# One more pass of two first-FFN blocks in groups of 15 block products, and nine weight sums made during the groups

## The chip, the cores and the metric

The kernel runs on one core of a Trainium2 chip. The metric is the device time of the whole program in microseconds. TensorE (PE) multiplies, VectorE (DVE) and ScalarE (ACT) work on SBUF and PSUM, GpSimd (POOL) on SBUF alone, and SyncE (SP) issues all the DMAs.

## What is computed

```python
# q, k, v, f_logit: 4 batches, 8 heads, 768 tokens, head_dim 48
f = 1 / (1 + exp(-f_logit))
for t in range(768):
    state = f[t][:, None] * state + outer(k[t], v[t])
    y[t] = q[t] @ state
x = y as 3072 tokens x 384
x = ((x @ w_a) * (x @ w_b)) @ w_out          # first FFN, d_ff 1536
p = domain_probs / (sum(domain_probs) + 1e-9)
out = sum over 4 experts e of p[:, e] * (relu(x @ w1[e]) @ w2[e])   # second FFN, d_ff 1024 each
```

## The kernel before

The 3072 tokens are eight blocks of TB1 = 384. Every float32 matmul is made from three: each operand is split into a rounded half (hi, made by ACT) and a rest (lo, made by VectorE or GpSimd), and hi x hi, lo x hi and hi x lo are added up in PSUM (`three`, L2577).

**Attention** is 32 units (a pair of heads, 384 tokens). Units 0 to 3 run alone at the start. Each of the others goes through limit, logs (exp and ln), sums (a scan), decays, inverses, ends, gates (GpSimd), keys, turn (transposes), krt, kv and scores (TensorE), mask and state (VectorE), output (TensorE) and y (ACT). The table `J` (L110) says at which part j of the plain FFN a unit's turn stands; the offsets of `TOGETHER` and its kin (L112) place its other steps. Units 8 to 31 are six parts apart.

**The first FFN, plain.** Blocks 0 to PLAIN - 1 = 5. One step i is one of 12 slices of d_ff of one block and has three parts: up_1(i, 0), up_1(i, 1) and down_1(i - 1), each of nine 384-column matmuls. ACT does a_out(i) and h_round(i), VectorE gate(i) and h_rest(i). Four loops over j in range(3 * N1) write out the order of TensorE, ACT, VectorE and GpSimd; SP has a fifth.

**Groups.** The other two blocks of the first FFN, and all of the second FFN, take two blocks (768 tokens) in a pass. The product of a 3 x 3 block matrix of weights (FG = 3 tiles of d_ff, 3 of d_model) with 3 x 2 blocks of x is made from 15 block products instead of 18 (`R`, `MADE`, `CHAINS`). For it, 11 sums of x blocks are made for each pass (x2_sum on VectorE, sum_hi on ACT, sum_lo on GpSimd), and 11 sums of weight blocks for each set of weights: w_sum(q, 0 to 15) on GpSimd, out of a buffer that load_w1(q) fills, and stored to DRAM by store_sums(q) (`weight_sums`). There are NS = 18 sets: 8 for the first FFN and 10 for the second. In a group, SP loads the set's 15 blocks (load_wu), ACT and GpSimd split them (up_round, up_rest), TensorE makes the products (up_2), ACT and VectorE copy and add the chains (copy, add), and h is made, split and multiplied down (h1_round, h1_rest or h2_round, h2_rest; down_round, down_rest; down) and added to the result (weigh). A pass of the first FFN is 8 groups, in turn one for a and one for b; a pass of the second is a small group of 2 tiles and ten full ones. The order inside a group is written out by hand for each engine; where passes change, three groups are written as one piece (`turned`, L534), since the next pass's x operands are made there.

All 18 weight sets are made during the plain blocks: w_sum(q) at parts SUMS_AT + SUMS_PACE * q (L163), with the loads and stores in SP's queue between the loads of the units. SP works its queue in order: an issue whose semaphore isn't there yet holds all that stand behind it. The buffer of x2_sum is a ring of NXT = 8 (2 for the first pass).

The lines that the prediction's steps touch: PLAIN (L40), `J` (L110), the sets' pace (L163), x2_sum's ring (L281, L1870), load_w1 (L791), store_sums, load_wd (L844), the SP loop over groups, turn (L2473), scores, kv and output, w_sum (L1522), product (L2695), down (L2779).

Of the kernel before, what the change touches and what calls it, by code (L numbers as in the profile page):

```python
# [7 lines left out]
def gated_attention_then_two_ffns(nc, fkq, v, vT, probs, wa, wb, wo, w1, w2, out):  # L8
# [31 lines left out]
    PLAIN = 6  # L40
# [10 lines left out]
    NS = 2 * NF + NQ  # L51
    TT = 2 * TB1 // 128
# [57 lines left out]
    J = {u: 5 * (u - FIRST) + 8 if u < 2 * PPB else 6 * (u - FIRST) + 5 for u in range(FIRST, NU)}  # L110
# [8 lines left out]

    FIRST_OF_2 = dict(CLOSE, logs=-7, sums=-6, decays=-5, ends=-4)  # L120
# [3 lines left out]
               for step, after in (FIRST_OF_2 if u == FIRST else SECOND_OF_2 if u == FIRST + 1 else LAST_OF_2 if u == 2 * PPB - 1 else CLOSE if u < 2 * PPB else  # L124
                                   LAST_OF_ALL if u == NU - 1 else TOGETHER).items()}
# [37 lines left out]
    SUMS_AT, SUMS_PACE = 31, 9  # L163
    WU_AT, WD_AT = (3 * FT1 * (PLAIN - 1) + 18, 3 * FT1 * (PLAIN - 1) + 32), 3 * FT1 * (PLAIN - 1) + 29

    def x2_at(n):
        return CMIN_AT + 9 + 2 * n
# [6 lines left out]
    with perm:  # L174
# [106 lines left out]
        NXT = 8  # L281
# [12 lines left out]

        for n in range(12, NX):
            x_operand(n)
# [378 lines left out]
        def x2_free(eng, p, o):  # L675
# [5 lines left out]
            elif n < 8 or n == 11:  # L681
                attention_done(eng)
            else:
                eng.wait_ge(s_upb, FT1 * (PLAIN - 1) + max(0, (n - 10) // 2))

# [25 lines left out]
        def w1_raw(f, k):  # L711
            return raw.rearrange("p a n -> p (a n)")[:, (k * FG + f) * 128:(k * FG + f + 1) * 128]
# [42 lines left out]
        def _(eng):  # L755
# [35 lines left out]
            def load_w1(q):  # L791
# [5 lines left out]
                dst = raw.rearrange("p a n -> p (a n)")[:, 0:KT * FG * 128].rearrange("p (k f) -> p k f", k=KT)  # L797
# [46 lines left out]
            def load_wd(g):  # L844
                if downs(g) == 0:
                    eng.wait_ge(s_ws, 16 * NS)
# [55 lines left out]
            for j in range(3 * N1):  # L902
# [14 lines left out]
                for q in range(NS):  # L917
                    if j == SUMS_AT + SUMS_PACE * q + 6:
                        if q + 1 < NS:
                            load_w1(q + 1)  # L920
                        store_sums(q)
                    if j == SUMS_AT + SUMS_PACE * q + 4:
# [9 lines left out]
            for g in range(G):  # L932
# [86 lines left out]
        def _(eng):  # L1019
            eng.preload_act_table_set("natural_log_exp_and_others")  # L1020

            def logs(u):
                t = unit_ring[ring(u)][0:P2, F, :]
                eng.wait_ge(s_lim, u + 1)
                eng.activation(t, t, ACT.Exp, scale=-1.0).then_inc(s_exp, 1)
                eng.wait_ge(s_exp, u + 1)
# [119 lines left out]

            logs(0)
            logs(1)
            decays(0)
            inverses(0)  # L1150
            decays(1)
            logs(2)
            inverses(1)
            logs(3)
# [23 lines left out]
            for j in range(3 * N1):  # L1178
                if j == STRONG_AT:
                    flag = is_strong(eng)  # L1180
                i, part = j // 3, j % 3
# [1945 lines left out]
```

## Time and profile before

| | |
|---|---|
| time, median of 3 runs | 1293.82 us (1293.12 to 1294.21) |
| the profiled execution | 1291.46 us, of it the span 1289.7 us |
| TensorE busy, matmul / weight load | 1280.1 / 1258.5 us |
| VectorE, ACT, GpSimd busy | 915.8, 635.5, 684.1 us |
| granted TensorE clock | 1.00 |

The stages by time: units 0 to 3 to about 28 us, plain blocks with attention to 380 us, plain blocks alone to about 440 us, the grouped pass of the first FFN to about 552 us, four passes of the second FFN to the end. "Busy" of an engine is the time covered by its instructions; a matmul's recorded 0.33 us overlaps the next one's. In the rows below, a time in brackets is how long the engine stood before the instruction, and the arrow names what let it go.

### The profile page before, as it was taken

To read this page: it belongs to the slowest core of one execution; us is meant where nothing else is said; L and a number is where in the kernel's file an instruction comes from. 1 tells how busy PE (TensorE), PEld (TensorE's weight loads), DVE (VectorE), ACT (ScalarE), POOL (GpSimd) and SP (SyncE) were. 2 spreads that over 40 slices of the span, in tenths; PEclk is the share of its full clock that TensorE was granted. 3 is DMA by queue.
4 is the path that set the end of the run, shared out by engine and by line. 5 is a ranking of instruction groups with operands and counts; after the bars stand their busy time and mean duration, and the time that the engine had idled before them with its cause. 6 is when DMAs were issued, how large, how long until landed. Compare 5 with 4: busy or idle time off the path is not lost.

```text
span 1289.7 us, 26428 instructions
## 1 busy us (share of the span) xinstructions
PE 1280.1 (99%) x9319; PEld 1258.5 (98%) x9319; DVE 915.8 (71%) x1775; ACT 635.5 (49%) x1316; POOL 684.1 (53%) x739
## 2 busy tenths in 40 slices
PE   9999999999999999999999999999999999999999
PEld 7999999999999989999999999999999999999998
DVE  8866766767645478767887677787668777677765
ACT  7654444445434455644444554445554455544442
POOL 4336766657656466574444744444744444644440
PEclk9999999999999999999999999999999999999999
DMA  8524445553433143132332242232342332432221
GB/s 258 171 75 147 138 137 153 157 163 117 130 98 128 56 124 93 61 109 87 98 99 81 83 145 83 86 99 61 104 137 85 98 92 66 138 110 87 82 86 38
DMA packets 90324, 140.59 MB, mean 109 GB/s; under 512 B 8848, under 2 KB 64336, under 8 KB 90192
## 3 DMA queue, kind: packets, MB, share of 16 engines
q1 hardware_dynamic: 90192, 138.89, 35.4%
q8 instruction: 76, 1.25, 0.4%
q14 instruction: 56, 0.46, 0.1%
HBM read 119.98 MB, written 22.41 MB: 110 GB/s over the span
## 4 chain that ended last, share of the span: by engine, by line
PE 97%; DVE 1%; DMA 0%; issue 0%; POOL 0%; ACT 0%; SPq 0%; DVEq 0%; ACTq 0%; POOLq 0%
PE bank L2809 10%; PE bank L2810 10%; PE bank L2808 10%; PE bank L2578 10%; PE bank L2580 9%; PE bank L2579 9%; PE bank L2708 6%; PE bank L2706 6%; PE bank L2707 6%; PE score_banks L2708 3%; PE score_banks L2706 3%; PE score_banks L2707 3%; PE bank L2568 2%; PE bank L2572 2%; PE score_banks L2497 1%; PE score_banks L2526 1%
## 5 line engine op out<-in xcount | busy, mean ns | idle before, releaser
L1576 POOL TENSOR_TENSOR wu<-w_r,wu 128x640 fp32r<-128x640 f32 (+1 forms) x156 | 242.4, 1568 | 96.2 <-ACT wu L1084 96.2
L1581 POOL TENSOR_TENSOR wd<-raw,wd 128x384 fp32r<-128x384 f32 x140 | 142.3, 1030 | 272.5 <-ACT wd L1089 272.5
L2120 DVE SCALAR_TENSOR_TENSOR xt<-bank,pn,xt 128x384 f32<-128x384 f32 x288 | 176.8, 615 | 148.7 <-PE bank L2810 143.9
L2808 PE MATMUL bank<-wd,h_hi 128*128 128x384 f32 x768 | 257.6, 335 | 0.0
L2809 PE MATMUL bank<-wd,h_hi 128*128 128x384 f32 x768 | 257.5, 335 | 0.0
L2810 PE MATMUL bank<-wd,h_lo 128*128 128x384 f32 x768 | 257.4, 335 | 0.0
L2708 PE MATMUL bank<-x_lo,wu 128*128 128x384 f32 x479 | 161.5, 337 | 0.0
L2706 PE MATMUL bank<-x_hi,wu 128*128 128x384 f32 x479 | 160.3, 335 | 1.0 <-DVE hb L2025 1.0
L2707 PE MATMUL bank<-x_hi,wu 128*128 128x384 f32 x479 | 160.3, 335 | 0.0
L2578 PE MATMUL bank<-xs_hi,wab 128*128 128x384 f32 x426 | 148.2, 348 | 0.4 <-ACT a_sb L1135 0.4
L2809 PEld LDWEIGHTS bank<-wd,h_hi 128*128 128x128 f32 x768 | 144.2, 188 | 0.0
L2808 PEld LDWEIGHTS bank<-wd,h_hi 128*128 128x128 f32 x768 | 144.2, 188 | 0.0
L2810 PEld LDWEIGHTS bank<-wd,h_lo 128*128 128x128 f32 x768 | 144.1, 188 | 0.0
L2579 PE MATMUL bank<-xs_hi,wab 128*128 128x384 f32 x426 | 142.7, 335 | 0.0
L2580 PE MATMUL bank<-xs_lo,wab 128*128 128x384 f32 x426 | 142.6, 335 | 0.0
L1105 ACT ACTIVATE h<-bank 128x384 f32<-128x384 f32 x144 | 67.6, 489 | 131.7 <-PE bank L2708 131.5
L1084 ACT ACTIVATE wu<-w_r 128x640 fp32r<-128x640 f32 (+1 forms) x156 | 105.7, 706 | 25.4 <-PE bank L2708 7.6
L2706 PEld LDWEIGHTS bank<-x_hi,wu 128*128 128x128 f32 x479 | 89.9, 188 | 1.4 <-DVE hb L2025 1.4
L2708 PEld LDWEIGHTS bank<-x_lo,wu 128*128 128x128 f32 x479 | 89.9, 188 | 0.0
L2707 PEld LDWEIGHTS bank<-x_hi,wu 128*128 128x128 f32 x479 | 89.9, 188 | 0.0
L1124 ACT ACTIVATE h_hi<-h 128x384 fp32r<-128x384 f32 x120 | 61.7, 521 | 45.3 <-DVE h L2045 42.2
L2578 PEld LDWEIGHTS bank<-xs_hi,wab 128*128 128x128 f32 x426 | 79.9, 188 | 2.6 <-ACT a_sb L1135 0.7
(253 smaller groups left out, 2871.5 us busy)
## 6 DMA issues: line engine op xcount, KB each, us to landing
w_r<-weight_sums SPq DMA_DIRECT2D x144, 320.0 KB, 2.9
raw<-w SPq DMA_DIRECT2D x48, 576.0 KB, 4.0
unit<-fkq SPq DMA_DIRECT2D x28, 504.0 KB, 4.6
weight_sums<-w_s SPq DMA_DIRECT2D x18, 384.0 KB, 4.5
v_in<-v_chunks SPq DMA_DIRECT2D x32, 144.0 KB, 4.2
out<-xt SPq DMA_DIRECT2D x24, 192.0 KB, 4.3
weight_sums<-w_s SPq DMA_DIRECT2D x54, 64.0 KB, 4.0
weight_sums<-w SPq DMA_DIRECT2D x40, 64.0 KB, 2.7
```

Of the source, the lines that this page charges most:

```text
L1576: eng.tensor_tensor(wu_piece(g, n, 1), wu_raw(g, n), wu_piece(g, n, 0).bitcast(f32), ALU.subtract).then_inc(s_ulo, 1)
L1581: eng.tensor_tensor(wd[half(g)][:, 1, n, :], wd_raw(n), wd[half(g)][:, 0, n, :].bitcast(f32), ALU.subtract).then_inc(s_dlo, 1)
L2120: eng.scalar_tensor_tensor(out=acc(b, t), in0=d, scalar=w, in1=acc(b, t), op0=ALU.mult, op1=ALU.add).then_inc(s_acc, 1)
L2578: eng.matmul(o, w_hi, m_hi, start=start, stop=False)
L2579: eng.matmul(o, w_lo, m_hi, start=False, stop=False)
L2580: return eng.matmul(o, w_hi, m_lo, start=False, stop=stop)
L2706: eng.matmul(to, w_hi, x_hi, start=start, stop=False, skip_group_check=True)
L2707: eng.matmul(to, w_lo, x_hi, start=False, stop=False, skip_group_check=True)
L2708: eng.matmul(to, w_hi, x_lo, start=False, stop=True, skip_group_check=True).then_inc(s_step, 1)
L2808: eng.matmul(o, hh, w_hi, start=(f == fs[0]), stop=False)
L2809: eng.matmul(o, hh, w_lo, start=False, stop=False)
L2810: mm = eng.matmul(o, hl, w_hi, start=False, stop=(f == fs[-1]))
```

## The change

- PLAIN goes from 6 to 4: blocks 4 to 7 of the first FFN are grouped, in two passes (groups 0 to 7 and 8 to 15); the groups of the second FFN are 16 to 59.
- The 28 later units of attention share 48 plain steps instead of 72. `J` spaces units 8 to 31 by 3.65 parts for SP; on the four other engines the loops over j are replaced by lists written out call by call. exps is taken out of logs, and exp and ln of a unit are placed apart.
- Sets 0 to 8 of the weight sums are made in the plain blocks (NSA = 9, pace 10), sets 9 to 17 in groups 2, 4, 6 to 8, 10, 14 to 16, 17, 18, 19 and 20, out of a new buffer raw_s. Its room comes from x2_t (NXT 8 to 5).
- load_w1 and store_sums for these sets stand in SP's loop over the groups, behind the group's load_wu and load_wd.
- scores waits for the states of the units before it, output(31) for the evacuation of unit 30.
- The order inside the groups is written anew, on all engines.

```diff
-    PLAIN = 6
+    PLAIN = 4
...
+    NSA = 9
...
-    J = {u: 5 * (u - FIRST) + 8 if u < 2 * PPB else 6 * (u - FIRST) + 5 for u in range(FIRST, NU)}
+    J = {u: 5 * (u - FIRST) + 8 if u < 2 * PPB else 29 + (u - 2 * PPB) * 365 // 100 for u in range(FIRST, NU)}
...
-    SUMS_AT, SUMS_PACE = 31, 9
+    SUMS_G = (2, 4, 8, 10, 14, 17, 18, 19, 20)
+    SUMS_AT, SUMS_PACE, SUMS_LONG = 31, 10, 8
...
-        NXT = 8
+        NXT = 5
...
+        raw_s = sb(later, "raw_s", [128, KT * FG * 128])
...
-            p, q = GROUPS[g]
-            after = 2 * NF if PASSES[p][0] == 1 else NQ
-            return q == after - 1 and p + 1 < len(PASSES) or q == NQ and p > 0
+            return any(r[0] < g <= r[-1] for r in ((14, 16), (6, 8), (25, 27), (36, 38), (47, 49)))
...
-                    eng.wait_ge(s_ws, 16 * NS)
+                    eng.wait_ge(s_ws, 16 * NSA)
...
+                if g + 1 in SUMS_G:
+                    q = NSA + SUMS_G.index(g + 1)
+                    if q > NSA:
+                        store_sums(q - 1)
+                    load_w1(q)
+                elif g == SUMS_G[-1]:
+                    store_sums(NS - 1)
...
+                    up_rest(g + 2, 2)
                     product(g + 1, 1)
                     product(g + 1, 2)
...
+                    for n in range(0, 4):
+                        w_sum(11, n)
                     sum_lo(p + 1, 6)
                     sum_lo(p + 1, 7)
                     sum_lo(p + 1, 8)
                     sum_lo(p + 1, 9)
                     sum_lo(p + 1, 10)
...
+                elif g == 18:
+                    up_rest(g + 1, 0)
+                    up_rest(g + 1, 1)
+                    up_rest(g + 1, 2)
+                    down_rest(g, 0)
+                    down_rest(g, 1)
+                    down_rest(g, 2)
+                    for n in range(0, 16):
+                        w_sum(15, n)
...
                 if u >= FIRST:
+                    eng.wait_ge(s_st, states(u, 0))
...
+                if u == NU - 1:
+                    eng.wait_ge(s_ys, NU - 1)
...
-            for j in range(3 * N1 - 2):
...
+            up_1(24, 1)
+            turn(20)
+            kv(20)
+            scores(20)
+            output(19)
+            down_1(23)
+            up_1(25, 0)
+            turn(21)
+            up_1(25, 1)
+            output(20)
+            kv(21)
...
```

## Rows read from the trace of the kernel before

**Rows 1.** The page's first part: busy time, share of the span, instructions of TensorE.
```profile
PE 1280.1 (99%) x9319; PEld 1258.5 (98%) x9319; DVE 915.8 (71%) x1775; ACT 635.5 (49%) x1316; POOL 684.1 (53%) x739
```
**Rows 2.** The page's chain of work that ended last, by engine.
```profile
PE 97%; DVE 1%; DMA 0%; issue 0%; POOL 0%; ACT 0%; SPq 0%; DVEq 0%; ACTq 0%; POOLq 0%
```
**Rows 3.** Stretches: length, then busy PE, PEld, DVE, ACT, POOL; clock, DMA, GB/s.
```profile
30.00:380.00 350.00, 349.30 (x3888) 332.82 (x3888) 235.54 (x487) 168.28 (x344) 208.49 (x329) 1.00 0.46 137
452.00:556.00 104.00, 101.10 (x578) 100.17 (x577) 80.04 (x158) 57.45 (x120) 66.66 (x54) 1.00 0.32 97
640.00:760.00 120.00, 120.00 (x692) 120.00 (x691) 88.43 (x167) 61.28 (x132) 64.81 (x54) 1.00 0.32 97
```
**Rows 4.** Timeline of PE, first groups: start, duration, instruction, [stood before it, releaser].
```profile
454.92 0.44 PE L2706 MATMUL bank<-x_hi,wu 128*128 128x384 f32 x1 [1.04 <-DVE hb L2025]
465.17 0.42 PE L2578 MATMUL bank<-h_hi,wd 128*128 128x384 f32 x1 [1.86 <-DVE h_lo L2073]
```
**Rows 5.** Timeline of PE in a full group, 27 matmuls apart.
```profile
700.15 0.33 PE L2808 MATMUL bank<-wd,h_hi 128*128 128x384 f32 x1
...
704.83 0.34 PE L2808 MATMUL bank<-wd,h_hi 128*128 128x384 f32 x1
```
**Rows 6.** The page's costliest groups: line, operation, count, busy us, mean ns.
```profile
L2808 PE MATMUL bank<-wd,h_hi 128*128 128x384 f32 x768 | 257.6, 335 | 0.0
```
**Rows 7.** Timeline of PE: output of two units in turn, and one turn.
```profile
161.72 0.86 PE L2568 MATMUL bank<-att,v_in 128*48 128x128 f32 x12
...
173.88 0.86 PE L2568 MATMUL bank<-att,v_in 128*48 128x128 f32 x12
...
205.17 0.45 PE L2481 MATMUL bank<-ident,kr 112*128 112x112 f32 x3
205.39 0.42 PE L2578 MATMUL bank<-xs_hi,wab 128*128 128x384 f32 x1
205.65 0.34 PE L2579 MATMUL bank<-xs_hi,wab 128*128 128x384 f32 x1
```
**Rows 8.** Timeline of ACT: the copy of a unit's transposes.
```profile
205.66 0.45 ACT L1046 ACTIVATE krt<-bank 128x336 f32<-128x336 f32 x1
```
**Rows 9.** h_rest and gate by line: count, duration ns min/median/max, first and last start.
```profile
L1862 DVE TENSOR_TENSOR h_lo<-h_sb,h_hi x72: 544/558/1941, 32.9 to 443.1; 128x384 fp32r<-128x384 f32 x72
L1858 DVE TENSOR_TENSOR h_sb<-a_sb,bank x72: 542/554/556, 31.1 to 441.9; 128x384 f32<-128x384 f32 x72
```
**Rows 10.** Two stretches of 10 us, columns as in rows 3.
```profile
40.00:50.00 10.00, 10.00 (x100) 9.62 (x99) 8.99 (x17) 7.61 (x14) 5.22 (x4) 1.00 0.78 225
50.00:60.00 10.00, 10.00 (x126) 9.50 (x125) 9.23 (x19) 6.20 (x12) 1.62 (x2) 1.00 0.38 112
```
**Rows 11.** Timeline of DVE: mask of a unit, first and last operation of its state.
```profile
200.54 1.22 DVE L1785 COPY_PREDICATED att<-causal,score_banks 64x384 f32<-64x384 int32 x2 [2.77 <-PE score_banks L2497]
...
204.68 0.20 DVE L1834 COPY st_in<-score_banks 112x48 f32<-112x48 f32 x1
...
206.12 0.26 DVE L1836 SCALAR_TENSOR_TENSOR st_carry<-st_in,cend,score_banks 112x48 f32<-112x48 f32 x1
```
**Rows 12.** Stretch, instructions that touch w_s alone: length, POOL busy (count).
```profile
30.00:380.00 350.00, 131.63 (x258) 1.00 0.46 137
```
**Rows 13.** up_rest, down_rest and sum_lo by line, columns as in rows 9.
```profile
L1576 POOL TENSOR_TENSOR wu<-w_r,wu x156: 733/1587/2002, 415.7 to 1249.1; 128x640 fp32r<-128x640 f32 x144, 128x256 fp32r<-128x256 f32 x12
L1581 POOL TENSOR_TENSOR wd<-raw,wd x140: 1003/1022/1379, 431.3 to 1264.2; 128x384 fp32r<-128x384 f32 x140
L1512 POOL TENSOR_TENSOR x_lo<-x_t,x_hi x55: 1004/1019/1336, 394.6 to 1108.4; 128x384 fp32r<-128x384 f32 x55
```
**Rows 14.** One issue of SP in the chain; DMA issues: count, KB each, us to landing.
```profile
1.28 0.42 SPq L767
...
raw<-w SPq DMA_DIRECT2D x48, 576.0 KB, 4.0
```
**Rows 15.** Waits: who for whom, us in total, times, longest.
```profile
POOL w_s L1535 <- DMA weight_sums<-w_s: 86.0, 17, 8.3
```

More of the change, by code:

```diff
@@ L118, in gated_attention_then_two_ffns @@
     LAST_OF_ALL = dict(TOGETHER, output=8, y=9, store=10)
+    NEAR = dict(load=-9, v=-4, limit=-6, logs=-5, sums=-5, decays=-4, gates=-3, ends=-3, keys=-2, turn=0, krt=1, scores=2, kv=2, mask=3, state=4, output=6, y=7, store=8)
     FIRST_OF_2 = dict(CLOSE, logs=-7, sums=-6, decays=-5, ends=-4)
@@ new lines, in _ @@
+            first_lo(9)
+            gate(4)
+            first_lo(10)
+            h_rest(4)
+            first_lo(11)
+            first_lo(12)
+            first_lo(13)
+            first_lo(14)
+            gate(5)
+            ends(6)
+            keys(6)
+            sums(7)
+            limit(8)
+            limit(9)
+            h_rest(5)
+            mask(5)
+            probs(0)
+            state(5)
+            ends(7)
+            sums(8)
+            first_lo(15)
+            gate(6)
@@ new lines, in _ @@
+            h_rest(6)
+            keys(7)
+            mask(6)
+            state(6)
+            ends(8)
+            first_lo(16)
+            sums(9)
+            keys(8)
+            gate(7)
+            mask(7)
+            state(7)
+            limit(10)
+            first_lo(17)
+            h_rest(7)
+            ends(9)
+            gate(8)
+            keys(9)
+            h_rest(8)
+            sums(10)
+            limit(11)
+            mask(8)
+            state(8)
+            ends(10)
@@ new lines, in _ @@
+            gate(9)
+            h_rest(9)
+            sums(11)
+            ends(11)
+            keys(10)
+            gate(10)
+            mask(9)
+            state(9)
+            h_rest(10)
+            gate(11)
+            h_rest(11)
+            keys(11)
+            probs(1)
+            limit(12)
+            limit(13)
+            mask(10)
+            gate(12)
+            state(10)
+            sums(12)
+            h_rest(12)
+            ends(12)
+            sums(13)
+            y_out_1(0)
@@ new lines, in _ @@
+            mask(11)
+            state(11)
+            gate(13)
+            limit(14)
+            h_rest(13)
+            keys(12)
+            gate(14)
+            ends(13)
+            sums(14)
+            keys(13)
+            ends(14)
+            h_rest(14)
+            mask(12)
+            state(12)
+            gate(15)
+            probs(2)
+            probs(3)
+            limit(15)
+            keys(14)
+            h_rest(15)
+            mask(13)
+            state(13)
+            limit(16)
@@ new lines, in _ @@
+            mask(21)
+            state(21)
+            ends(23)
+            keys(23)
+            h_rest(26)
+            mask(22)
+            state(22)
+            gate(27)
+            sums(24)
+            h_rest(27)
+            mask(23)
+            state(23)
+            limit(25)
+            gate(28)
+            limit(26)
+            ends(24)
+            keys(24)
+            h_rest(28)
+            sums(25)
+            sums(26)
+            ends(25)
+            keys(25)
+            mask(24)
@@ L2019, in add @@
+            x2_sum(0, 9)
+            gate(46)
+            plain_lo(0, 3)
+            x2_sum(0, 10)
+            h_rest(46)
+            gate(47)
+            h_rest(47)
+            flag = is_strong(eng)
             def add(g, n):
```

2060 lines of the change are left out of this document (1527 added, 533 removed).

## Prediction

> **What bounds the kernel now.** I read the page from the top. TensorE is busy for 1280.1 of 1289.7 us [rows 1], and the chain that ended last runs through it for 97% of the span [rows 2]. So the time is the number of matmuls times their distance, plus the few places where TensorE stands. The table of stretches says where those are: from 30 to 380 us (attention beside the first FFN's plain blocks) TensorE stands 0.7 us, from 640 to 760 us not at all, and from 452 to 556 us (the one pass of grouped first FFN) 2.9 us, the others at start and end [rows 3]. The 2.9 us are two single waits: 1.04 us before the fifth product of group 1, for an add, and 1.86 us before the first down product of group 1, for h_lo [rows 4]. VectorE and GpSimd are far from full in these stretches, 67% and 60% in the attention stretch, 77% and 64% at most in the groups [rows 3]. They can't shorten anything, but they can become late.
>
> **Matmuls removed.** A matmul of 384 columns starts 4.68 us / 27 = 0.1733 us after the one before it [rows 5], at a granted clock of 1.00 (the level of 2.4 GHz) in every stretch of rows 3, in the groups and in the plain blocks alike; I use 0.1735 us. A plain block has 12 steps of up_1 (a and b, 3 k, 3 halves: 18) and down_1 (3 tiles, 3 halves: 9), so 324 matmuls, and two blocks 648. The same two blocks as one pass of groups: 8 groups of 15 products of 3 matmuls, 360, and 4 down parts of 6 tiles, 3 f and 3 halves, 216, together 576. 72 matmuls less: 72 x 0.1735 = **12.5 us** off TensorE. The second FFN keeps all of its own, among them the 3 x 768 of its down products [rows 6].
>
> The Trainium skill, "TensorE: Matmul & The Clock Gate", section "Back-to-back issue gap", gives N/2.4 + 2.5 ns for an isolated gap, 162.5 ns at 384 columns, and the saving by it would be an estimated 11.7 us. The same section says that streams with weight loads do better than that at 512 columns; rows 5 show worse than the formula at 384 columns and the rule is not borne out here.
>
> **Attention, moved closer together.** The 28 later units used to be spread over 58 of 72 steps; the order written out now ends with output(31) after up_1(39, 0), 522 matmuls or 90.6 us sooner. Their own matmuls stay. A unit costs TensorE 173.88 - 161.72 = 12.16 us less 54 x 0.1735, so 2.8 us [rows 7]. A switch to small matmuls and back loses time: the three transposes at 205.17 take 0.22 us to the next weight-heavy matmul, which in turn is followed after 0.26 us and not 0.17 [rows 7]. I put a switch at 0.1 to 0.15 us. Before there are 58 such switches after the first four units; in the new order I count 49, since turn(u + 1) often stands right behind scores(u). 9 x 0.11 = **1.0 us** saved; bounds 0 and 1.5.
>
> Against this stand new waits. One is written in: turn(20) is followed at once by kv(20), which needs ACT's copy of the transposes. The copy takes 0.45 us [rows 8], and with a hop before and behind it TensorE stands **0.8 us** (bounds 0.45 and 1.2), and nothing else is queued to cover it. In all other units at least a down_1 or an up_1 (1.56 us) lies between the two.
>
> The other is VectorE's load. From 30 to 380 us it is busy 235.5 us [rows 3]. 58.5 steps of gate and h_rest at 2 x 0.55 us [rows 9] are 64 us, the splits of late weights and probs some 13, and the rest is 28 units at 5.6 us. Now the same 28 units share 350 - 91 = 259 us with 19.3 steps less: 235.5 - 21 = 214 us, so 83% of the stretch, up from 67%. It is uneven. Between gate(25) and gate(29) VectorE has four units and four steps, 22.4 + 4.4 = 26.8 us, and TensorE has 108 matmuls and three units, 18.7 + 8.4 = 27.1 us: 99%. Between gate(5) and gate(9) it is about as full, with seven weight and unit items in front. Between gate(29) and gate(37) it falls to 70%. In the old kernel VectorE ran 90% and 92% full in two slices of 10 us with TensorE at 10.00 of 10.00 [rows 10], so high load alone costs nothing there. At 99% it does; I take **1.5 us**, bounds 0 and 8.
>
> The round trip is what makes it sharp. output(u) waits for mask(u) and state(u), 1.22 us and 1.7 us on VectorE [rows 11], 2.9 us together, counted from scores(u). Before, six parts of a step (9.4 us) lay between scores and output. In the new order seven units (6, 7, 12, 15, 21, 24, 27) have only turn and two parts, 3.6 us, and five more have 4.4 to 4.6 us. The slack of such a unit is 0.7 us, and whatever VectorE is late beyond that TensorE waits.
>
> **Weight sums moved.** A set is 16 GpSimd operations. 258 of them take 131.6 us [rows 12], so a set is 8.2 us. Nine of 18 sets leave the plain blocks and go into groups 2 to 20, into a buffer of their own, raw_s, whose room comes from x2_t (8 buffers to 5). GpSimd has room in the first of these: two groups of the first FFN are 144 matmuls or 25 us, and hold six up_rest at 1.59, three down_rest at 1.02 [rows 13] and two products of about 1.05, so 14.7 us, 22.9 with a set. In groups 17 to 20 (99 matmuls, 17.2 us) it holds 7.8 + 8.2 = 16.0 us: 93%. The sums stand last in each list, and up_rest of the next group is wanted a whole group later, so I cost them at nothing. If that cover goes, each us of lateness is a us.
>
> At one place the cover seems too short. At the pass change of groups 6 to 8, w_sum(11, 0 to 3) stands ahead of sum_lo(6 to 10). Its data comes by load_w1(11), which SP issues only after load_wu(9) and load_wd(9) and the five stores of set 10, behind up_rest(8, 2). Eight issues of 0.42 us and a landing of 4.0 us [rows 14] are 7.4 us after up_rest(8, 2); GpSimd has two products (2.1 us) to do meanwhile and then stands with five sum_lo behind the wait. Counted from the start of group 7: up_rest(8, 2) ends at about 11.9 (1.0 until the first piece is there, three up_rest 4.8, six sum_lo 6.1 [rows 13]), the data is there at 19.3, sum_lo(6) ends at 22.3. Group 8's ninth product, which reads it, stands after 15 + 8 products and 5 down tiles, 114 matmuls or 19.8 us. TensorE stands **2.5 us**; bounds 0 and 4. In the old kernel GpSimd waited 86 us in 17 places for such stores and loads, up to 8.3 us [rows 15], none of it felt by TensorE, which speaks for the lower bound.
>
> The two waits of rows 4 stay: the lines of group 0 on ACT and of TensorE around group 1 are the same (y_out and three up_round ahead of copy(1, 0)). I cost the reorder at nothing, bounds -2 and +1. The pass change that is new (first FFN to first FFN) is three groups of 36 us; 30 adds, 11 sums, 4 plain_lo and some 17 other operations at 0.5 us are 31 us on VectorE, 86%, and I put it at nothing, bounds 0 and 2. New waits before scores (s_st) and before output(31) are for things that kv and the order have waited for already: nothing.
>
> **Sum.** -12.5 - 1.0 + 0.8 + 1.5 + 2.5 = -8.7 us. The profiled execution took 1291.46 us, so 1282.8 by it; the median of the runs is 2.36 us above it, so **1285.1 us**.
>
> **Rivals.**
> (a) The whole gain: the lists hide everything but kv(20), and one wait of group 1 goes. -12.5 - 1.0 + 0.8 - 1 = -13.7: 1280. For it: in the groups of the old kernel, which are written out in the same manner, TensorE never stands from 640 to 760 us [rows 3].
> (b) VectorE is the bound in the two full stretches. Its operations with two SBUF inputs stretch beside GpSimd: h_lo has 558 ns as the median and 1941 at most, while h_sb, with one input in PSUM, never exceeds 556 [rows 9]. With more packed into less time 27 us at 99% become 110%, twice or three times: 6 to 8 us more than I took, 1291. The Trainium skill, "SBUF — State Buffer", section "Who interferes with whom", has the pair of ports as an exclusive lock: by that rule the second to come waits a whole instruction. Rows 9 agree.
> (c) GpSimd is late in the groups: at 93%, with its operations stretched by the same contention (640-wide ones to 2002 ns [rows 13]), groups 17 to 20 and the two pass changes lose about 1.5 us each: 9 us on top of none from the attention, 1290.
> (d) Slower: the round trip scores, mask, state, output sets the pace of the attention. With two units in flight a late mask delays output, evacuation and the next turn. It decides against the change from 13.5/28 = 0.48 us of standing per unit on; at 0.65 us per unit it is 18 us and 1298. For it: a slack of 0.7 us in seven units. Against it: units with 8 to 15 us of room stand between, in which VectorE catches up.
>
> **Chances.** Forecast (1282 to 1288) 0.45; (a) 0.21; (b) 0.12; (c) 0.08; (d) 0.14. A measurement of this kernel can tell 0.2%, or 2.6 us. (b) and (c) end at 1288 to 1295, a little over half of them below 1291.2, so faster 0.77, same 0.09, slower 0.14. The range reaches over (a), (b) and (c), from 1279.0 to 1295.0, and leaves (d) out.
>
> **What would show it.** The count of 384-column matmuls down by 72. TensorE's idle time by stretch: under 1 us from 640 us on; up to 3 us before up_2(8, 8) with GpSimd at w_sum waiting for a DMA; 0.8 us at kv(20), with ACT's krt as releaser; a few tenths at L1785 or L1836 as releasers where units come in pairs. (b) would show as masks or gates as releasers around gate(5 to 9) and gate(25 to 29); (c) as up_rest or sum_lo; (d) as state before most outputs. Wrong altogether would be a longer distance of matmuls, or a clock below 1.00 after new waits.

## The result and the profile after

The kernel after takes 1362.87 us (median of 4 runs, 1353.32 to 1364.68), the kernel before 1293.47 us beside it (1292.65 to 1294.21). The ratio is 1.052, 95% interval 1.047 to 1.057: **5.2% slower**, where 1285.1 us was forecast, and 68 us beyond the top of the range.

The page's first part, and the chain of work that ended last, of after:

```profile
PE 1298.8 (95%) x9247; PEld 1267.3 (93%) x9247; DVE 971.8 (71%) x1884; ACT 662.5 (49%) x1373; POOL 723.7 (53%) x788
...
PE 68%; POOL 5%; issue 2%; DMA 2%; DVE 2%; SPq 1%; ACT 1%; DVEq 0%; ACTq 0%; POOLq 0%
```

TensorE has 9247 matmuls where it had 9319 [rows 1]: the 72 are gone, as counted. Yet it is busy 18.7 us longer and stands 64.2 us of the span of 1363.0, where it stood 9.6. The chain went through TensorE for 97% [rows 2], now for 68%. Three stretches of after, with the columns of rows 3:

```profile
30.00:330.00 300.00, 270.30 (x3263) 249.74 (x3267) 193.84 (x437) 136.94 (x294) 127.18 (x193) 0.95 0.42 122
360.00:700.00 340.00, 313.19 (x1720) 307.44 (x1719) 247.08 (x438) 161.81 (x336) 249.91 (x294) 0.96 0.38 118
700.00:1300.00 600.00, 600.00 (x3453) 600.00 (x3452) 450.53 (x844) 306.69 (x632) 297.20 (x243) 1.00 0.32 97
```

The attention stretch holds 29.7 us of standing, the groups in which weight sums are made 26.8 us, and behind 700 us there is none. VectorE is busy 65% in the first and 73% in the second: idle time of TensorE beside idle time of VectorE means that both wait. The granted clock was 0.95 and 0.96, where it was 1.00 everywhere in rows 3. Six of the larger stands (one of 4.68 us, at 69.50, is the largest of the attention), from TensorE's timeline (start, duration, instruction, [stood before it, releaser]), and two of the waits (who for whom, us in total, times, longest):

```profile
206.56 0.66 PE L3442 MATMUL bank<-h_hi,wo_hi 128*128 128x384 f32 x1 [4.35 <-DVE h_lo L2390]
...
441.79 0.69 PE L3805 MATMUL score_banks<-x_hi,wu 128*128 128x384 f32 x1 [2.46 <-DVE hb L2831]
...
487.15 0.69 PE L3805 MATMUL score_banks<-x_hi,wu 128*128 128x384 f32 x1 [3.55 <-DVE h L2831]
...
533.72 0.59 PE L3805 MATMUL score_banks<-x_hi,wu 128*128 128x384 f32 x1 [3.49 <-DVE hb L2831]
...
634.69 0.69 PE L3805 MATMUL score_banks<-x_hi,wu 128*128 128x384 f32 x1 [6.06 <-DVE h L2867]
...
689.47 0.44 PE L3907 MATMUL bank<-wd,h_hi 128*128 128x384 f32 x1 [3.21 <-DVE xt L2926]
```
```profile
DVE unit L2249 <- DMA unit<-fkq: 45.0, 18, 6.5
...
POOL w_s L1882 <- DMA raw_s<-w: 30.0, 4, 8.8
```

**The sum.** By my working TensorE should have stood 9.6 us plus 0.8 + 1.5 + 2.5 = 14.4 us, and been busy 1280.1 - 12.5 - 1.0 = 1266.6 us. It stood 64.2 (+49.8) and was busy 1298.8 (+32.2). These 82.0 us are the difference between the span of the profiled execution, 1363.0 us, and the 1281.0 us that the working gives for one.

**The busy time** grew mostly because TensorE ran at the lower of its two clock levels (1.2 GHz) about its longer stands. Its timeline behind the stand of 2.46 us:

```profile
442.59 0.52 PE L3807 MATMUL score_banks<-x_lo,wu 128*128 128x384 f32 x1
442.91 0.52 PE L3805 MATMUL bank<-x_hi,wu 128*128 128x384 f32 x1
443.23 0.52 PE L3806 MATMUL bank<-x_hi,wu 128*128 128x384 f32 x1
...
445.14 0.34 PE L3806 MATMUL bank<-x_hi,wu 128*128 128x384 f32 x1
445.32 0.34 PE L3807 MATMUL bank<-x_lo,wu 128*128 128x384 f32 x1
```

Matmuls of 384 columns start 0.32 us apart and, some 3 us later, 0.18. At full clock it is 0.1733 [rows 5]; ten of them at 0.32 cost 1.5 us more. The granted clock of after was 0.50 in twelve stretches, eight of 3.4 us and four of 6.8, and TensorE was busy for 49.5 us in them. By an estimate from that, half of those 49.5 us, 24.8, is the most that the clock can have cost of the 32.2.

The other 7.4 us or more have another cause. The kernel mended (experiment 10) has 3.4 us at the lower level and is still busy for 1277.1 us, only 3.0 less than before, where the working had 13.5 less. A stand costs busy time beyond its own length: the last matmul ahead of it counts its whole 0.33 us, of which the next one otherwise overlaps 0.16, and the first one behind it comes 0.28 us before the next and not 0.17. TensorE stands for 0.05 us or more in 8 places before, in 43 in after and in 37 in mended. At 0.27 us each that is some 9 and 8 us, an estimate which no run here tests.

**The attention.** Where does VectorE wait? Before 206.56 its timeline has limit(u), which takes the logits of a unit, and h_lo, which TensorE wants, right behind it:

```profile
205.52 0.36 DVE L2249 TENSOR_SCALAR unit<-unit 112x384 f32<-112x384 f32 x1 [3.58 <-DMA unit<-fkq]
205.79 0.16 DVE L2268 COPY cend<-dec 112x6 f32<-112x6 f32 x1
205.87 0.55 DVE L2390 TENSOR_TENSOR h_lo<-h_sb,h_hi 128x384 fp32r<-128x384 f32 x1
```

The data is late, and VectorE, which works its list in order, can't go past it. When was it asked for? The end of output(u - 4) on TensorE, SP's issue of the next unit, and limit, in one of the cases:

```profile
212.91 0.22 PE L3436 MATMUL bank<-unit,st_in 48*48 48x64 f32 x2
...
213.17 0.34 SPq L766 DMA_DIRECT2D unit<-fkq  x1
...
217.86 0.36 DVE L2249 TENSOR_SCALAR unit<-unit 112x384 f32<-112x384 f32 x1 [0.52 <-DMA unit<-fkq]
```

The issue comes 0.26 us behind the last matmul that reads the old unit, the data 4.7 us after it. A unit's buffer is one of a ring of four, and load(u) waits for s_y of unit u - 4. Units are 3.65 steps apart, so y(u - 4) stands at J(u) - 14.6 + 7 = J(u) - 7.6, behind the step written for the load, -9. A step takes 1.56 us of plain matmuls and 2.8 / 3.65 us of a unit's, about 2.3 us without any stand. So the 4.7 us are 2.0 steps, the data is there at about -7.6 + 2.0 = -5.6 at the best, and limit(u) stands at -6. In the kernel before the same sum was -24 + 10 = -14 against a limit at -10: 4 steps of room. That is my theory of the ring, found only after the first experiments.

### The profile page after: what moved, and what is told of

Read it like the earlier page. It is cut to its first block, busy times and chain, and to the rows that moved or that the text cites. A ratio compares the mean times of both kernels' runs of the same rounds, so it can differ in the third digit from the quotient of the medians.

```text
span 1363.0 us, 26767 instructions
## 1 busy us (share of the span) xinstructions
PE 1298.8 (95%) x9247; PEld 1267.3 (93%) x9247; DVE 971.8 (71%) x1884; ACT 662.5 (49%) x1373; POOL 723.7 (53%) x788
## 4 chain that ended last, share of the span: by engine, by line
PE 68%; POOL 5%; issue 2%; DMA 2%; DVE 2%; SPq 1%; ACT 1%; DVEq 0%; ACTq 0%; POOLq 0%
PE bank L3909 10%; PE bank L3908 10%; PE bank L3907 10%; PE bank L3807 6%; PE bank L3805 6%; PE bank L3806 6%; PE score_banks L3805 3%; PE score_banks L3807 3%; PE score_banks L3806 3%; PE bank L3442 3%; PE bank L3444 3%; PE bank L3443 3%; POOL wu L1923 2%; DMA raw_s<-w 1%; SPq L833 1%
## 5 line engine op out<-in xcount | busy, mean ns | idle before, releaser
L1928 POOL TENSOR_TENSOR wd<-raw,wd 128x384 fp32r<-128x384 f32 x152 | 154.5, 1029 | 320.7 <-ACT wd L1108 320.7
L1923 POOL TENSOR_TENSOR wu<-w_r,wu 128x640 fp32r<-128x640 f32 (+1 forms) x180 | 277.1, 1563 | 24.1 <-ACT wu L1103 24.1
L3805 PE MATMUL bank<-x_hi,wu 128*128 128x384 f32 x559 | 190.0, 340 | 4.4 <-DVE hb L2831 1.5
L3807 PE MATMUL bank<-x_lo,wu 128*128 128x384 f32 x559 | 190.2, 340 | 0.0
L3806 PE MATMUL bank<-x_hi,wu 128*128 128x384 f32 x559 | 189.0, 338 | 0.0
L1103 ACT ACTIVATE wu<-w_r 128x640 fp32r<-128x640 f32 (+1 forms) x180 | 122.6, 709 | 70.1 <-PE bank L3807 30.0
L3805 PEld LDWEIGHTS bank<-x_hi,wu 128*128 128x128 f32 x559 | 106.9, 191 | 7.0 <-DVE hb L2831 2.2
L3805 PE MATMUL score_banks<-x_hi,wu 128*128 128x384 f32 x281 | 96.1, 342 | 17.2 <-DVE h L2867 6.8
L3442 PE MATMUL bank<-xs_hi,wab 128*128 128x384 f32 x282 | 101.8, 361 | 10.2 <-DVE h_sb L2386 5.1
L3806 PEld LDWEIGHTS bank<-x_hi,wu 128*128 128x128 f32 x559 | 106.6, 191 | 0.0
L3807 PEld LDWEIGHTS bank<-x_lo,wu 128*128 128x128 f32 x559 | 106.5, 190 | 0.0
L3443 PE MATMUL bank<-xs_hi,wab 128*128 128x384 f32 x282 | 98.2, 348 | 0.0
L3444 PE MATMUL bank<-xs_lo,wab 128*128 128x384 f32 x282 | 97.9, 347 | 0.0
```

The source lines that it names most:

```text
L1923: eng.tensor_tensor(wu_piece(g, n, 1), wu_raw(g, n), wu_piece(g, n, 0).bitcast(f32), ALU.subtract).then_inc(s_ulo, 1)
L1928: eng.tensor_tensor(wd[half(g)][:, 1, n, :], wd_raw(n), wd[half(g)][:, 0, n, :].bitcast(f32), ALU.subtract).then_inc(s_dlo, 1)
L3442: eng.matmul(o, w_hi, m_hi, start=start, stop=False)
L3443: eng.matmul(o, w_lo, m_hi, start=False, stop=False)
L3444: return eng.matmul(o, w_hi, m_lo, start=False, stop=stop)
L3805: eng.matmul(to, w_hi, x_hi, start=start, stop=False, skip_group_check=True)
```

## Experiments

Thirteen kernels. "Standing" is TensorE's in 30:330 and in 360:700; after has 29.7 and 26.8. Experiments 4, 10 and 13 are medians of four runs, all others single runs. The four runs of after lie 11.4 us apart and those of experiment 4 12.9 us, so where two times differ by less than that, the stands in the traces have to tell.

**1. no_sums**: leaves out every weight sum with its loads, copies and stores; the groups multiply by blocks of w1 in place of the sums.

> Leaves out all weight sums with their loads, copies and stores, in the plain blocks and in the groups (the groups multiply by blocks of w1 instead, so the result is not the reference's). Changed kernel: 1363 us, TensorE stands 30 us from 30 to 330 us and 27 us from 360 to 700 us, and works at a lower granted clock behind the stands, some 31 us more of busy time. Theory 1 (queue order): unit loads are late since SP issues sum copies and stores ahead of them, and in the groups up_rest is late since GpSimd's w_sum stands before it waiting for a load: standing falls to under 10 us in the attention stretch and under 5 us in the groups, time 1285 to 1300. Theory 2 (VectorE is the bound at 99% in the full stretches): the attention stretch keeps over 20 us of standing, time 1315 to 1330. Theory 3 (ring of four unit buffers): the same as theory 2 for the attention.

Measured: 1310.97 us, clock 0.996, standing 14.1 and 9.6; VectorE still waits 22.1 us for unit data. So about 52 of the 69 us over before come with the sums, in both stretches, and 17 do not (theory 1 had 1285 to 1300, theory 2 over 20 us of standing: neither came). With no sum at all this kernel is slower than the old one with all of them.

**2. groups_sums_last**: the sums of sets 9 to 13 behind all up_rest and down_rest of a group and none where passes change; load_w1 one group earlier, ahead of the stores.

```
-    SUMS_G = (2, 4, 8, 10, 14, 17, 18, 19, 20)
+    SUMS_G = (1, 3, 5, 9, 11, 13, 17, 18, 19)
...
-                elif g == 4:
-                    for n in range(0, 4):
-                        w_sum(10, n)
-                    up_rest(g + 1, 0)
...
+                elif g in (2, 4, 10, 12):
...
+                    for n in range(8):
+                        w_sum({2: 9, 4: 10, 10: 12, 12: 13}[g], n)
```

> Weight sums 9 to 13 stand behind the up_rest and down_rest of their group on GpSimd, none in the pass changes, and SP issues load_w1 ahead of the five stores of the set before. All else as in the changed kernel. Theory 1 (in the groups GpSimd's list waits for raw_s with up_rest behind it): standing from 360 to 700 us falls from 27 to under 8 us and its share of low clock goes, time 1325 to 1340. Rival (GpSimd's load itself, 16 operations more per set, makes it late): standing stays above 18 us, time above 1350.

Measured: 1342.78 us, standing 28.0 and 13.1, between what the two theories gave. The stands of 2.46 and 3.49 us are gone. So is the one of 3.21 us, and the one of 6.06 is 1.92: these two have a cause of their own, below. This is their chain in after (start, duration, what), for the first of them:

```profile
420.22 0.48 SPq L833
...
424.00 0.45 SPq L815
424.50 4.96 DMA raw_s<-w
429.53 0.46 POOL w_s L1882
...
431.25 1.54 POOL wu L1923
...
433.77 3.09 POOL wu L1923 x2
436.92 2.96 DMA w_r<-weight_sums
440.60 0.48 ACT hb L1124
441.18 0.57 DVE hb L2831
```

SP stores set 9 in five issues, then loads set 10; GpSimd has w_sum(10, 0 to 3) written ahead of up_rest(5, 0) and waits for the load; up_rest is late, so the raw block's buffer, so the next load of blocks, so TensorE.

**3. units_by_act** and **4. both_orders**: ScalarE issues the loads of units 10 to 31 and of v right behind evac_y(u - 4), past SP's queue; 4 has the edit of 2 as well.

```
+            unit_from(eng, 10)
+            v_from(eng, 10)
```

> Units 10 to 31 and their v are loaded from ACT's queue right behind evac_y of the unit that frees the buffer, units 8 and 9 earlier in SP's queue. Groups as in the changed kernel. Theory 1 (loads behind other issues of SP): VectorE's waits for unit data fall from 45 to under 15 us, standing from 30 to 330 us from 30 to under 12 us, time 1320 to 1335. Theory 2 (VectorE is the bound): waits fall but standing stays over 20 us. Theory 3 (four buffers are too few): waits stay over 25 us since the data is asked for at the same output, standing stays over 20 us.

> Both edits together. Theory 1: little standing anywhere, the clock stays at 1.00, and the 72 matmuls show: 1283 to 1295, about 1288, faster than the kernel before by up to 0.8%. Theories 2 or 3 for the attention: 1310 to 1330.

Measured: 1359.73 us, standing 28.1 and 27.9; and 1342.67 us (ratio 1.038, 1.033 to 1.043), standing 29.3 and 16.4. VectorE waited 37.0 and 34.2 us for the data. The theory that SP's long runs of issues made the loads late fell: another queue, and no gain. What both kernels keep is that the load follows output(u - 4).

**5. forget_rows_first**: limit(u) takes only the logits of a unit, and its buffer's row of logits is read for the last time by the key gate, nine steps before output. The row gets a transfer of its own:

```
+            def load_gates(u):
+                eng.wait_ge(s_kg, before_in_ring(u) + 1)
+                eng.dma_start(unit_ring[ring(u)][0:P2, F, :], fkq[pair_of(u), half_of(u), :, F, :])\
+                   .then_inc(s_f[ring(u)], 16)
```

> The kernel after, but from unit 6 on the forget rows of a unit (which limit(u) takes) are loaded by a transfer of their own, as soon as the key gate of unit u-4 has read that row; the key and query rows follow as before, behind output(u-4). One more transfer for each unit on SyncE's queue, the order of every other engine unchanged. Theory ring (limit(u) waits because the unit's buffer is given back only by output(u-4), and its transfer takes 4.5 us more, while the written order has limit(u) 3 steps behind the load): VectorE's wait for unit data falls from 45.0 us to under 10, TensorE's standing in 30:330 from 29.7 us to 10 to 15, time about 1340. Theory VectorE (the shorter spacing simply gives VectorE and the loop scores, mask, state, output too little time): the wait for data falls too, but TensorE stands as before, 25 to 30 us, time 1355 to 1365.

**6. both_and_forget_rows**: with the order of 2 (not 4: the loads stay with SP).

> The same loads with the order of the weight sums in the groups of groups_sums_last. If the two faults are separate, their gains add: theory ring gives 1342.78 less about 20, so some 1320, with 28.0 us of standing in 30:330 falling to 10 to 15; theory VectorE gives 1340 to 1345.

Measured: 1349.1 and 1318.93 us. In 5, wait and stretch:

```profile
DVE unit L2262 <- DMA unit<-fkq: 12.1, 5, 4.4
...
30.00:330.00 300.00, 281.98 (x3446) 260.74 (x3447) 217.10 (x461) 147.43 (x315) 141.57 (x213) 0.99 0.47 134
```

The wait falls from 45.0 to 12.1 us, the standing from 29.7 to 18.0, the clock rises from 0.95 to 0.99, with no order of a computing engine changed. In 6 the standing is 12.1 and 16.3. The gains are 13.8 and 20.1 alone and 43.9 together: 10 us more than their sum, which three single runs against runs 11.4 us apart suggest and do not show. The theory of the ring holds for the 11.7 us of standing (15.9 from experiment 2 to 6), and the rival that VectorE has too little time explains at most what is left. The standing stayed above the 10 to 15 us expected of 5; one of its stands, 3.38 us at 180.29, follows a limit that lasted 6.52 us beside weight sums (below).

**7. no_sums_ring_five**: the kernel of 1 with a fifth buffer and loads at step -11.

> The kernel no_sums (no weight sums, no load, copy or store of them) with a fifth buffer for units from unit 11 on, laid over the region in which the weight sums had their raw weights, and unit loads two steps earlier (at -11). Theory ring: in no_sums VectorE still waited 22.1 us for unit data and TensorE stood 14.1 us in 30:330; with data there early the wait falls under 5 us, the standing to 5 to 9 us, and the time from 1310.97 to about 1304. Theory VectorE: the standing stays at 12 to 15 us and the time at 1310.

Measured: 1310.54 us, standing 10.9 and 10.6; the wait for data falls from 22.1 to 9.3 us. The wait and the standing did not fall as far as expected (under 5 us, and 5 to 9), and the time is the one that the rival gave. Over the whole span TensorE stood 3.2 us less and was busy 2.7 us more (1280.6 for 1277.9), with 13.7 us at the lower clock level for 10.2. So this pair alone does not decide between the two theories. The largest stand left, 3.80 us at 68.6, is that of units 8 and 9, which no later buffer serves.

**8. stands_put_into_before**: TensorE waits in the middle of five full groups for 1, 2, 3, 1 and 5 tiny transfers in turn.

```
+                if g in STANDS and n == 7:
+                    eng.wait_ge(s_stand, 16 * stands_before(g))
```

> The kernel before, with TensorE made to wait in the eighth block product of groups 24, 27, 35, 38 and 46 for 1, 2, 3, 1 and 5 tiny transfers of SyncE one after the other, nothing else changed. It prices a stand of TensorE by itself, with what the granted clock does behind it. Theory clock (the low clock behind a stand is what made TensorE's busy time 31 us longer in the kernel after): stands of 4 us and more are followed by 384-column matmuls 0.32 us apart instead of 0.173 for some us, so that the kernel is longer by clearly more than the sum of the stands, while the short ones cost their own length. Rival (the low clock of the kernel after has another cause, its transfers or its many short idle times): each stand costs its own length, some 2 us for each transfer, 24 us together, and the clock stays at 1.00.

Measured: 1324.98 us, 30.9 over before, with 23.3 us of stands. Stretches (columns as in rows 3) with a stand of one transfer, of two, and behind that of five:

```profile
815.00:825.00 10.00, 7.95 (x46) 7.67 (x46) 5.75 (x11) 2.56 (x6) 4.41 (x4) 1.00 0.31 100
869.00:879.00 10.00, 6.22 (x27) 5.93 (x26) 3.53 (x7) 1.36 (x3) 4.32 (x4) 0.83 0.30 99
...
1212.00:1222.00 10.00, 9.33 (x45) 9.36 (x46) 4.76 (x9) 2.29 (x5) 0.00 (x0) 0.81 0.29 98
```

The two stands of about 2.0 us cost their length and the clock stays at 1.00. Behind 3.78 us, and behind the two longer ones, TensorE runs for 3.2 us at half the clock (ten matmuls at 0.32 us), and then at the full one: 1.5 us each. But the length of a stand does not settle it. The same trace has such a stretch of ten matmuls at two places where nothing was put in, behind stands of 1.66 and 1.85 us:

```profile
31.20 0.58 PE L2589 MATMUL bank<-xs_hi,wab 128*128 128x384 f32 x1 [1.66 <-ACT a_sb L1146]
...
467.89 0.41 PE L2589 MATMUL bank<-h_hi,wd 128*128 128x384 f32 x1 [1.85 <-DVE h_lo L2084]
```

The second of them is the 1.86 us of rows 4, behind which before stayed at full clock. Against the traced run of before (1291.46 us) the kernel is 33.5 us longer: TensorE stands 24.3 us more and is busy 9.3 us more, of which five stretches of ten slow matmuls are 7.5.

**What a run of GpSimd does to VectorE.** In after, two instructions of VectorE lasted 8.27 and 4.12 us. The first, its neighbours, and GpSimd's first and last sum at that time:

```profile
623.99 0.54 DVE L2855 TENSOR_TENSOR h<-h,score_banks 128x384 f32<-128x384 f32 x1
624.46 8.27 DVE L2872 SCALAR_TENSOR_TENSOR h_lo<-h,h_hi 128x384 fp32r<-128x384 f32 x1
632.64 0.55 DVE L2859 TENSOR_TENSOR bank<-h,bank 128x384 f32<-128x384 f32 x1
```
```profile
626.02 0.50 POOL L1882 TENSOR_TENSOR w_s<-raw_s 128x128 f32<-128x128 f32 x1
626.44 0.49 POOL L1884 TENSOR_TENSOR w_s<-raw_s 128x128 f32<-128x128 f32 x1
...
632.38 0.65 POOL L1919 TENSOR_TENSOR w_s<-w_s,raw_s 128x128 f32<-128x128 f32 x1
```

From 620.99 GpSimd goes from one instruction to the next, the sums (sixteen) 0.42 us apart, up to the last, which waits for the one before it and starts 0.07 us behind its end. There VectorE comes in. The Trainium skill, "SBUF — State Buffer", section "Who interferes with whom", says that a VectorE instruction with two SBUF inputs and a GpSimd instruction that reads SBUF exclude each other, and that the loser waits until the other finishes. The trace shows the same pair of instructions, but a wait through 17 GpSimd instructions and not one.

Nor is it confined to two inputs or to the groups. In forget_rows_first limit(u), which reads one tile in SBUF and took 0.36 us above, lasts through a weight sum of the attention, and again up to the gap before the sum's last instruction (VectorE's line, and GpSimd's first, last but one and last):

```profile
171.64 6.52 DVE L2262 TENSOR_SCALAR unit<-unit 112x384 f32<-112x384 f32 x1
...
171.67 0.47 POOL L1893 TENSOR_TENSOR w_s<-raw 128x128 f32<-128x128 f32 x1
...
177.49 0.46 POOL L1927 TENSOR_TENSOR w_s<-w_s,raw 128x128 f32<-128x128 f32 x1
178.03 0.92 POOL L1930 TENSOR_TENSOR w_s<-w_s,raw 128x128 f32<-128x128 f32 x1
```

**9. after_sums_with_gaps**: every weight sum waits for the one before it.

```
+                else:
+                    eng.wait_ge(s_ws, 16 * q + n)
```

> The kernel after; every weight sum on GpSimd now waits for the one before it, so that GpSimd's queue has a gap of some 0.1 us between two of them. Nothing else moves. In the trace of after two VectorE instructions of line 2872 (h_lo from two operands in SBUF, 0.55 us elsewhere) last 8.27 and 4.12 us while GpSimd runs weight sums one right behind the other, and TensorE stands 6.06 and 3.21 us behind them. Theory access (GpSimd's unbroken run keeps VectorE from an operand; a gap lets it in): no VectorE instruction of that line over 2 us between 400 and 700, the stands of 6.06 and 3.21 us gone or under 1 us, each weight sum about 0.1 us longer, time about 1350. Rival (the long record is something else, such as the weight sums' transfers): the long instructions stay and the time is 1360 to 1365.

Measured: 1351.4 us, 11.5 less, which is about as far as the runs of after lie apart. The longest of these instructions between 400 and 700 us are now 3.03 and 2.12 us; of the stands of 6.06 and 3.21 us 0.83 is left. By these stands the theory of access holds, if less purely than I wrote (no such instruction over 2 us).

**10. mended**: 6 with the gaps, with the forget rows of units 8 and 9 ahead of store_x(4), and with this order of ScalarE where passes 0 and 1 change:

```
                     copy(g + 2, 0)
-                    copy(g + 2, 1)
                     h1_round(g + 1, 2)
                     plain_hi(p + 1, 3)
+                    h1_round(g + 1, 3)
...
+                    copy(g + 2, 1)
```

> The kernel both_and_forget_rows with three more edits: every weight sum waits for the one before it; the forget rows of units 8 and 9 are loaded at steps 11 and 12, ahead of the six copies of store_x(4); at the first change of passes ScalarE makes h1_round(7, 2 to 4) and three operands before copy(8, 1) and not behind it. Four stands of TensorE in both_and_forget_rows belong to these: 3.21 us at 67, 3.55 at 454, 2.27 at 607 and 3.45 at 644. By my theories all four go, 12.5 us, and with them some 1.7 us of low clock behind each of three: 1318.9 - 12.5 - 5 = about 1301. If the low clock behind stands were not theirs, 1306; if the third theory is wrong, 1310 or more. The rest to the kernel before would be the small stands of TensorE in the attention.

Measured: **1307.14 us** (ratio 1.011, 1.009 to 1.012), clock 0.998:

```profile
30.00:330.00 300.00, 292.33 (x3516) 271.77 (x3517) 214.53 (x470) 150.44 (x323) 154.93 (x218) 0.99 0.47 138
...
360.00:700.00 340.00, 330.23 (x1881) 325.98 (x1880) 268.12 (x494) 173.41 (x358) 267.02 (x298) 1.00 0.41 131
```

Three of the four stands are gone and the one of 3.55 us is 1.40. 11.8 us came of the 17.5 expected. 55.7 of the 69.4 us by which after is slower are found, each by an edit that moves no work away.

**11. bursts_put_into_before**: sixteen small GpSimd instructions behind down_rest(g, 2) of five late groups; **12. bursts_like_sums**: the same kind of thing in the mended kernel, with the weight sums' own instructions too.

> The kernel before, with 16 small GpSimd instructions added behind down_rest(g, 2) in five full groups: in groups 24 and 35 additions 128x128 of two tiles in SBUF one right behind the other, in 27 and 46 the same with a wait for the one before each, in 38 memsets of 128x128. It shows what a run of GpSimd instructions by itself does to VectorE. Theory access: in 24 and 35 a VectorE instruction with two operands in SBUF lasts several us, until the run ends, and TensorE stands behind it for 2 to 6 us each; in 27 and 46 none is longer than about 1.5 us and TensorE does not stand; in 38 none, as a memset reads nothing. Time 1298 to 1306. Rival (GpSimd's later weight halves are what delays, not VectorE's access): all five groups look the same, and the time is within 2 us of before.

> The kernel mended, with 16 GpSimd instructions added in six full groups behind 700 us: in groups 29, 40 and 43 the sixteen instructions of a weight sum again (operands in the loaded weights, results over the sums, waits as in the kernel after), behind the last, the middle and ahead of the first down_rest; in 32 the same with a wait for the one before each; in 34 and 45 the additions of bursts_put_into_before. Theory access, in the form that is left (an unbroken run keeps VectorE out only at the pace of a weight sum, 0.42 us from start to start, not at the 0.48 us that the additions took): in at least one of 29, 40 and 43 a VectorE instruction with both operands in SBUF lasts over 2 us, up to the end of the run, and none in 32, 34 and 45; time 1308 to 1325. If none is long in any group, the long instructions of the kernel after have a condition that these runs do not name, and it stays open; time about 1307.

Measured: 1292.57 us, and no instruction of VectorE over 2 us: this miss says that a run of GpSimd alone isn't enough. In 12, 1327.42 us, with four of them, the first two in a run of sums (group 29) and in one of additions (group 34):

```profile
780.80 5.56 DVE L2922 SCALAR_TENSOR_TENSOR h_lo<-h,h_hi 128x384 fp32r<-128x384 f32 x1
...
869.99 4.50 DVE L2922 SCALAR_TENSOR_TENSOR h_lo<-h,h_hi 128x384 fp32r<-128x384 f32 x1
```

TensorE stands 2.32 to 3.41 us behind each. Groups 29, 34, 43 and 45 have one; 40 has none, nor has 32, whose instructions wait for each other. In 45 the additions were over and it lasted beside the group's own up_rest and down_rest. So the kind of GpSimd's instructions doesn't decide. Their pace doesn't either: in 11, too, the additions start 0.42 us apart, and the 0.48 us that I had expected to matter is a mean over the run, in which those beside VectorE's two-input instructions took 0.78 us. There VectorE got in between two of them:

```profile
821.11 7.71 POOL L1634 TENSOR_TENSOR w_s<-w_s 128x128 f32<-128x128 f32 x16
...
821.62 0.78 DVE L2084 SCALAR_TENSOR_TENSOR h_lo<-h,h_hi 128x384 fp32r<-128x384 f32 x1
```

In after (8.27 and 4.12 us) and in 12 the long instruction is h2_rest(g, 1), the first h_lo of its group whose operands are both in SBUF, but the limit above is no such instruction. What makes VectorE wait for the end of the run in one case and get in between in the other stays open.

**13. mended_output_earlier**: output(u) one step earlier on TensorE.

> The kernel mended with output(u) one step earlier in TensorE's loop for units from 8 on (step 5 and not 6 behind turn(u)), all written lists unchanged. The copies of y(u-2), which turn(u) waits for, then end before turn(u) is there. Theory loop (the six stands of 0.48 us at turn(u) follow from output(u-2) standing right ahead of turn(u), since units are 3.65 steps apart): these stands go, 2.9 us, and the time falls from 1307.14 to about 1304. Rival (VectorE's state(u) and mask(u) have no slack): output(u) now waits for VectorE, new stands come in place of the old ones, and the time is 1307 or more.

Measured: 1308.08 us (ratio 1.011). The stands of 0.48 us stayed, since ScalarE's copy kept its place, and a new one of 2.00 us came, with VectorE's gate as its releaser. The rival was right: here, at the end, VectorE and the round trip have no room left, as (d) said, but for 4.4 us of standing in the attention (12.1 for 7.7) and not for 18.

## Why the prediction was wrong

**Right.** The 72 matmuls. kv(20): 0.54 us of standing with krt as releaser, for 0.8 forecast. The two old waits, 1.04 and 1.77 us here for 1.04 and 1.86 [rows 4]. Nothing behind 640 us but for weight sums. A clock below 1.00 as a sign that it is all wrong; I had named it and given it no price.

**Step 1, unit loads, absent from the sum.** The new waits before scores and before output(31) were weighed (at nothing), but not the load that moved from -14 to -9 with its wait for y(u - 4). All of its numbers were there: a ring of four, 3.65 steps, a landing of 4.6 us on the old kernel's page (4.7 in after). The old kernel's trace had a small sign: VectorE's wait for unit data, 4.7 us in 5 places, of which two of 0.7 us lie behind 100 us, with 4 steps of room. This and the list of VectorE that puts limit(u) ahead of gate and h_rest is 11.7 of the 29.7 us by experiment 5, and 15.9 of 28.0 between 2 and 6; VectorE's term (1.5 us, bounds 0 and 8) priced load, and it is busy 65%, not 83%.

**Step 2, weight sums in the groups: "I cost them at nothing".** That "the sums stand last in each list" is wrong for groups 4, 6, 10 and 14, where they are written ahead of up_rest or sum_lo. I worked the place out once, for w_sum(11), 2.5 us with bounds 0 and 4. The stand that is there, 3.55 us at 487.15, isn't its doing: no_sums has it too (3.55 us at 456), and ScalarE's order removes most of it. The 2.46 and 3.49 us are at w_sum(10) and w_sum(12), which wait for their load with up_rest behind them, and for which I did no such working. With all sums left out (experiment 1) 52 of the 69 us are gone.

**Step 3, rival (b).** It had VectorE's instructions stretched "a whole instruction" by GpSimd's, from rows 9 with 1941 ns at most. The maximum of the old kernel was no bound: the stretch is as long as GpSimd's unbroken run. It cost 9.3 us of standing at two places of after, both in the groups and neither in the attention, where I looked. In forget_rows_first it is there too, and one input in SBUF was enough for it.

**Step 4, the busy time: -12.5 - 1.0.** The count of matmuls was right and the 13.5 us were not: TensorE is busy 18.7 us longer, 32.2 over the working. At most 24.8 of these are the lower clock, which was in none of my cases and adds 1.0 to 2.5 us (7 to 17 matmuls at 0.32 us) to a stand. The rest, and 9 us or so in mended, I had put at nothing without a reason; by the estimate above it is the overlap of matmuls that each new stand breaks. For the 1.0 us of fewer switches no run here shows a gain.

**The order written out and the bounds.** Every rival was costed as one cause among causes that do not meet. But a late limit makes later outputs, later loads and later limits, and experiments 2, 5 and 6 (43.9 us together against 33.9 apart) suggest that two such faults cost more together.

**Open.** 13.7 us between mended and before, 27 to the whole gain of (a). By the two profiles TensorE stands 26.1 us for 9.6 and is busy only 3.0 us less. Of the mended kernel's profile 7.7 us are standing in the attention (six times 0.48 us at turn(u), for ScalarE's copy of y(u - 2), and single ones under 0.7), some 7 us in the first FFN's second pass, whose change of passes is new (0.85, 1.06, 1.40, 1.58, 0.82, 1.49), and 1.4 us more at the first gate. No version here beats the kernel before.

## What to carry to other kernels

When iterations are moved closer together, recompute every ring: the step at which its buffer comes back, plus the landing time, against the step of the first reader, and not only the engines' load. Where engines work written lists, an early step that waits for a transfer holds everything behind it; give its operand a transfer of its own if it is free sooner than the rest. Price a stand of TensorE with what the lower clock can take behind it (here up to 2.5 us, and about it already at stands of 1.5 to 2.2 us in some cases), and look in the trace for VectorE instructions stretched beside a long unbroken run of GpSimd; a wait before each of its instructions cut that from 8.27 to 3.03 us here.

## What the hardware showed that was not expected

All eleven stands of after of 2.2 us and more have a stretch at the lower clock level about them, and so has one of 1.53 us (at 30.97), while one of 1.77 us (401.49) has none. In other kernels stands of 3.27 us (units_by_act, 130.33) and 3.14 us (forget_rows_first, 69.05) passed at full clock. The stand ahead of the first down product of the groups, 1.75 to 1.93 us in every kernel here, went either way: at full clock in before and in mended, with ten slow matmuls in stands_put_into_before. So length alone doesn't decide, and from 1.5 to 3.3 us both happen. The lower level lasted 3.4 or 6.8 us in after, with 7 to 17 matmuls at 0.32 us; in some cases it began only after TensorE was running again (1.4 us after, behind the stand of 3.21 us). The Trainium skill, "TensorE: Matmul & The Clock Gate", section "Wait — 56ns, not 53.3ns?", gives N / 1.2 GHz from start to start at the lower level, 320 ns at 384 columns; the 0.32 us here agree.

A VectorE instruction with two SBUF operands took 8.27 us beside 17 GpSimd instructions of 0.5 to 1.0 us each, fifteen times its own 0.55 us, and one with a single SBUF operand 6.52 us. It came in where GpSimd's instruction waited for the one before it, a gap of 0.07 us, and with such a wait before each sum the longest was 3.03 us.
